# Three orders changed and one bank added in the expert tiles of an attention, MLP and mixture-of-experts kernel

## What is computed

```python
logits = xn @ en.T / tau
expert_idx = np.argmax(logits, axis=1)
...
for e in range(E):
    mask = expert_idx == e
    h = np.maximum(x[mask] @ w1[e], 0.0)      # 512 -> 1024
    out[mask] = gate_w[mask, None] * (h @ w2[e])  # 1024 -> 512
```

## Time and profile before

| | us |
|---|---|
| median of 3 runs | 981.75 (981.25 to 981.96) |
| profiled execution, device time | 981.86 |
| its span, first to last instruction | 979.9 |
| TensorE busy / its weight loads busy | 956.0 / 792.8 |
| VectorE, ScalarE, GpSimd busy | 577.8, 255.2, 239.2 |
| mean granted TensorE clock | 0.998 |

### The profile page before, as it was taken

The page is one execution under the profiler, slowest core; times in us unless marked ns, Lnnn a source line. Parts: engine busy times, 40 slices in busy tenths (PEclk is TensorE's granted clock), DMA queues, the critical chain, the costliest instruction groups (busy, mean ns, idle before and its releaser), DMA issues.

```text
span 979.9 us, 16519 instructions
## 1 busy us (share of the span) xinstructions
PE 956.0 (98%) x5444; PEld 792.8 (81%) x5445; DVE 577.8 (59%) x1078; ACT 255.2 (26%) x404; POOL 239.2 (24%) x192
## 2 busy tenths in 40 slices
PE   8999999999999999999999999999999999999996
PEld 7888888888888888888887888878788788787785
DVE  4656589647964697469845987664333632423531
ACT  4222121112111111121111312332433533323531
POOL 4443123331433142414341224120000000000000
PEclk9999999999999999999999999999999999999999
DMA  8431392033002300140012123355331451423311
GB/s 287 166 131 55 119 386 101 0 115 101 0 0 86 128 0 0 47 146 1 1 44 93 70 87 110 105 169 220 129 130 52 181 225 43 170 82 116 113 41 53
DMA packets 27121, 100.47 MB, mean 103 GB/s; under 512 B 4383, under 2 KB 4767, under 8 KB 22448
## 3 DMA queue, kind: packets, MB, share of 16 engines
q1 hardware_dynamic: 19280, 80.90, 23.2%
q0 software_dynamic: 4336, 12.61, 3.3%
q10 hardware_dynamic: 3456, 6.32, 2.3%
HBM read 87.19 MB, written 24.20 MB: 114 GB/s over the span
## 4 chain that ended last, share of the span: by engine, by line
PE 90%; issue 3%; DVE 2%; ACT 2%; ACTq 1%; DMA 1%; SPq 0%; DVEq 0%; POOL 0%; POOLq 0%
PE bank L676 27%; PE bank L694 27%; PE bank L801 13%; PE bank L769 11%; PE bank L572 2%; PE bank L784 2%; PE bank L618 2%; PE bank L588 2%; ACT weights_split L1370 1%; PE bank L605 1%; PE bank L661 1%; DMA en_all<-in_qk 1%; DVE attention L887 1%; DVE en_all L1138 0%; ACT scratch L1399 0%
## 5 line engine op out<-in xcount | busy, mean ns | idle before, releaser
L676 PE MATMUL bank<-activations_split,weights_split 128*128 128x512 f32 x1152 | 277.6, 391 | 0.4 <-issue 0.4
L694 PE MATMUL bank<-weights_split,activations_split 128*128 128x512 f32 x1152 | 276.1, 389 | 0.0
L694 PEld LDWEIGHTS bank<-weights_split,activations_split 128*128 128x128 f32 x1152 | 216.1, 188 | 44.9
L676 PEld LDWEIGHTS bank<-activations_split,weights_split 128*128 128x128 f32 x1152 | 215.1, 188 | 45.9 <-issue 1.5
L1511 POOL TENSOR_TENSOR activations_split<-scratch,activations_split 128x512 fp32r<-128x512 f32 x84 | 116.9, 1391 | 327.2 <-ACT activations_split L1290 319.8
L1290 ACT CAST activations_split<-scratch 128x512 fp32r<-128x512 f32 x96 | 59.8, 623 | 412.1 <-DVE scratch L927 412.1
L801 PE MATMUL bank<-weights_split,activations_split 128*128 (+1 forms) x648 | 161.5, 398 | 2.8 <-issue 1.8
L769 PE MATMUL bank<-weights_split,activations_split 128*128 (+1 forms) x648 | 153.3, 391 | 0.1
L769 PEld LDWEIGHTS bank<-weights_split,activations_split 128*128 128x128 f32 x648 | 121.0, 188 | 25.2 <-issue 0.5
L801 PEld LDWEIGHTS bank<-weights_split,activations_split 128*128 128x128 f32 x648 | 117.8, 188 | 26.4 <-issue 2.6
L986 DVE SCALAR_TENSOR_TENSOR attention<-rows,en_all 128x512 f32<-128x512 f32 x140 | 135.0, 1005 | 0.0
(11 more groups left out here) (183 smaller groups left out, 667.1 us busy)
## 6 DMA issues: line engine op xcount, KB each, us to landing
attention<-in_w_exp SPq DMA_DIRECT2D x24, 1024.0 KB, 4.9
attention<-in_kv SPq DMA_DIRECT2D x43, 256.0 KB, 3.7
expert_rows<-in_pad_rows SPq DMA_DIRECT2D x8, 1028.0 KB, 18.4
en_all<-in_w_exp SPq DMA_DIRECT2D x8, 1024.0 KB, 7.2
rows<-in_w_mlp SPq DMA_DIRECT2D x14, 512.0 KB, 3.3
rows<-expert_rows ACTq DMA_DIRECT2D x24, 257.0 KB, 2.9
attention<-in_qk SPq DMA_DIRECT2D x12, 512.0 KB, 4.7
scratch<-in_qk SPq DMA_DIRECT2D x10, 512.0 KB, 3.7
```

Source lines behind the costliest of these rows:

```text
L676: last = mm(H_ps[f % 2][:, :], win(a, kc, f), x[:, kc, :], start=(k == 0), stop=(k == 3 * KC - 1))
L694: last = mm(bank[j][:, :], x[f % 2][:, j * P:(j + 1) * P], wout(a, f), start=(f == 0 and a == 0 and part_ == "hi"), stop=(f == FB - 1 and ...
```

## The change

It has four parts. (1) In each tile VectorE does its ReLU half ahead of `w1_part`. (2) ScalarE issues `load_rows` for tile t+3 behind `x_hi_part(t+2)` and no longer at the head of the tile. (3) `expert_down` alternates between banks 2 and 3, and waits for the result copy of tile t-2; tile 0 waits for none, and tile 1 waits for the last rank result in bank 3 to be read (`s_rk`). (4) At the start VectorE does `h_lo_part(0, 0)` and `relu_half(1)` in one go, and only then the tile table's last three pieces.

```diff
-    XT_ps, EH_ps, HT_ps, EY_ps = bank[6], [bank[4], bank[5]], [bank[0], bank[1]], bank[2]
+    XT_ps, EH_ps, HT_ps, EY_ps = bank[6], [bank[4], bank[5]], [bank[0], bank[1]], [bank[2], bank[3]]
@@ expert_down, TensorE
-                pe.wait_ge(s_yd, due(s_yd, t))
+                if not (isinstance(t, int) and t < 2):
+                    pe.wait_ge(s_yd, due(s_yd, t - 1))
+                elif isinstance(t, int) and t == 1:
+                    pe.wait_ge(s_rk, due(s_rk, NC))
...
-                        last = mm(EY_ps[:, :], x[tt % 2][:, fc * P:(fc + 1) * P],
+                        last = mm(EY_ps[tt % 2][:, :], x[tt % 2][:, fc * P:(fc + 1) * P],
@@ the tile table, VectorE
+            h_lo_part(0, 0)
+            relu_half(1)
             link(ve.tensor_tensor(past[o], bc(const("tile")[o, :], E), over_tiles(t_end), ALU.is_ge))
...
             link(ve.tensor_copy(tab[o, T_EXP:T_EXP + TILES], eid[o, 1:TILES + 1]))
-            h_lo_part(0, 0)
...
             link(ve.tensor_scalar(tab[o, T_ROW:T_ROW + TILES], row_f[o, :], row_first[o, 0:1], float(PAD), ALU.add, ALU.min))
-            relu_half(1)
@@ tile, VectorE
                 e_next = next_expert(t + 1)
+                relu_half(t + 1)
                 w1_part(e_next)
-                relu_half(t + 1)
                 x_lo_part(t + 2, tt + 2)
@@ y_part, ScalarE
-                se.activation(y_sb[tt % 4], EY_ps[:, :], ACT.Copy, scale=tail[:, 0:1]).then_inc(s_yd, 1)
+                se.activation(y_sb[tt % 4], EY_ps[tt % 2][:, :], ACT.Copy, scale=tail[:, 0:1]).then_inc(s_yd, 1)
@@ tile, ScalarE
                 t = 4 * i + tt
-                if not (isinstance(t, int) and t == 2):
-                    load_rows(act, i, tt + 3)
                 e_next = next_expert(t + 1)
                 w1_part(e_next, t)
                 relu_half(t + 1)
                 x_hi_part(t + 2, tt + 2)
+                if not (isinstance(t, int) and t == 2):
+                    load_rows(act, i, tt + 3)
                 w2_part(e, t)
```

## The result

| | before | after |
|---|---|---|
| median (range), us | 981.63 (981.25 to 981.96) | 969.70 (969.37 to 970.04) |
| span of the profiled execution, us | 979.9 | 968.0 |
| ratio of the times | | 0.9877, 95% interval 0.9865 to 0.9889 |

The kernel became 11.9 us faster; the forecast was 970.3 us, in a range of 969.0 to 973.5.

What follows compares the result with a forecast made beforehand. TensorE, busy for 98% of the span, was taken as the bound, so only its gaps could be won. 8.6 (loop stalls) + 1.6 (start) + 1.3 (end) = 11.5 us off 981.75 gave 970.3 us, range 969.0 to 973.5.

Steps and rivals of the forecast that it cites:

- The bound and part 1: In the loop, VectorE's ReLU half ahead of the weights ends six TensorE stalls at the ReLU transposes: 8.6 us.
- up to 1.3 us a time: At the tile head, ScalarE's first cast starts earlier without the row load; worth this alone, nothing beside part 1.
- The cover of 0.69 us: Row split's low part ends at T+5.89, TensorE wants it at T+6.58; T is the start of a tile's row transposes.
- Parts 3 and 4, the end: At the start 1.6 us of 2.8 are left; at the last tile 1.3 us, between 1.15 and 1.41.
- SP's chain: At the start, SP's row load for tile 4 lands at 666.08, so TensorE waits until about 666.15.
- (a): In the loop, the cover is gone and TensorE waits before `up`, 1.8 to 4.8 us in all: 972 to 975; 12%.
- (b): The ReLU transposes wait for something other than VectorE's order; only parts 3 and 4 count: 978.9 us; 4%.
- (c): In the loop, row loads take over 10.1 us to land, TensorE waits 20 times; at 10.8 us, 984.3; 4%.
- (d): In the loop, something outside TensorE (GpSimd's scatter or SP) takes the gains back: 981.7 us; 2%.

Runs made afterwards that it cites:

- e1: Part 1 alone (VectorE's ReLU half in front of the weights) on the kernel before: 972.37 us, ratio 0.9908.
- e4: The changed kernel with part 2 undone (ScalarE's row load at the head of the tile again): 969.71 us.
- e3: The changed kernel with part 1 undone (VectorE's ReLU half behind `w1_part` again): 970.45 us.
- e7: The changed kernel with one extra VectorE ReLU into an unused buffer ahead of the ReLU half, tiles 2 to 23: 971.84 us.
- e8: The changed kernel with three extra VectorE ReLUs into unused buffers ahead of the ReLU half, tiles 2 to 23: 978.95 us.
- e5: Part 3 alone (two result banks and their waits) on the kernel before: 980.25 us, ratio 0.9986.
- e12: The changed kernel with two of the eight pads issued by ScalarE instead of SP: 968.90 us, ratio to before 0.9869.
- e9: The changed kernel with ScalarE's row load moved behind the result copy at the tile's end: 987.62 us, ratio to before 1.0054.
- e10: The changed kernel with four of the eight pads issued by SP ahead of the wait for the tile table: 974.04 us.
- e11: The changed kernel with five of the eight pads issued by SP ahead of the wait for the tile table: 974.49 us.

## Why the prediction was right

**The bound and part 1.** As worked out: the stalls at the ReLU transposes were the order on VectorE, and six waits of 8.6 us in sum are gone (e1). Missed was the gap of 0.5 us at the loop head behind tile 15, which goes with them.

**Part 2.** "Nothing" beside part 1 is what e4 shows. Its worth alone, "up to 1.3 us a time", was right in size (8.0 us for six). The prediction did not say what follows from that: part 1 is worth only 0.9 us beside part 2 (e3). Its sum gave the 8.6 us to part 1; they belong to either.

**The cover of 0.69 us.** The thinnest place was named rightly, and its size was wrong: 0.18 us. VectorE was 0.1 later than counted (T+5.99 for T+5.89). And the prediction read the time at which TensorE wants the row split from the start of its weight load in a stream without a stall, T+6.58; by e7 and e8 it is 0.40 earlier. The term was too large by 0.5 us, and that it held was luck: 0.2 us more work on VectorE would have begun to cost. The branch between ReLU and subtractions cost nothing, as taken: the subtractions start 0.60 us after the ReLU does, the same distance as from the ReLU to the row split before.

**Parts 3 and 4, the end.** The last tile waits for nothing now. By the table under e3 and e4 that gave 1.2 us (e5 against before; the change against e1 gives 1.1), where 1.3 was forecast and 1.15 was the lower bound. The row transposes of tile 4 wait on SP's chain for 1.2 us, where 1.1 was forecast, and begin at 666.12 where 666.15 was. The start thus gave 667.76 - 666.12 = 1.6 us. That this chain bounds it is shown by e12, which shortened it and took that wait from 1.2 to 0.2 us.

**The sum.** 11.5 forecast, 11.9 measured: 9.1 for 8.6, 1.6 for 1.6, 1.2 for 1.3. The loop head's 0.5 is the main difference.

**The rivals.** (a) did not happen. e7 and e8 show that it was closer than its price assumed: with a cover of 0.18 us a stall of 1 us would have cost 0.8 a time. (b) fell with e1. (c) needs the late place of e9. Its price was 14 us for 20 equal waits; in e9 it was five waits in the loop, 14.3 us in sum, and about 3 us more from the clock, which the prediction did not count. It also had the row loads "mostly ahead of the weight pieces"; they mostly are, but one took 8.6 us. (d) fell with the result.

## What to carry to other kernels

When two engines in a row delay the same instruction, moving either one can clear the wait, and the gains of the two moves do not add: price each of them beside the other before giving a gain to one. The deadline of an operand is not where its consumer's first instruction starts in a smooth stream, but earlier, by all that its sequencer does between the wait and that instruction. An engine that stands idle at the start of a phase is no free place for a transfer as long as others wait for transfers that are in flight then. A long wait of TensorE can cost more than its length: look at the granted clock behind it.

## What the hardware showed that was not expected

At a loop head without a stall in front, TensorE's second table read began about 2 us ahead of the product that needs it (830.1, 832.18); with a stall right in front it was 1.1 us (838.5, 839.59), and the weight loads stood idle for 0.5 us. From the end of VectorE's operand to TensorE's next weight load it took 0.40 us where address registers and a second semaphore followed (e7, e8), and 0.06 us where nothing followed. Four pads of 257 KB within HBM, issued beside four row scatters, went with a landing time of these of 6.8 us instead of 2.9 (e10). Behind waits of 3.3 to 4.1 us TensorE's granted clock fell to 0.50 for more than 2 us in some cases (e9 twice, e11) and stayed at 1.00 in others (e9 twice, e10); behind the six waits of 1.6 us in e8 it did not fall (0.99 to 1.00).
